# Attention with split operands and a two-stage MLP on one core: transposed tiles in single banks of PSUM, the inverses spread as a row through DRAM, the first weight tiles split on GpSimd, and new orders on every engine

## The reference

```
h = x @ w_in;  r = max(h, 0);  y = (s * r * r + b) @ w_out           # first
h = y @ w2_in; y2 = (h * sigmoid(1.702 h)) @ w2_out                   # second
```

## Time and profile before

| | |
|---|---|
| median of 3 runs | 1165.56 us |
| profiled execution: its own time, its span | 1168.41 us, 1166.6 us |
| busy in the span: TensorE, VectorE, ScalarE, GpSimd | 95%, 47%, 44%, 20% |
| attention, up to the first matmul of the MLP | 355.48 us |
| the rest, the two MLPs | 811.1 us |
| mean granted clock of TensorE | 0.996 of full |

### The profile page before, as it was taken

The page is one execution under the profiler, slowest core; times in us unless marked ns, Lnnn a source line. Parts: engine busy times, 40 slices in busy tenths (PEclk is TensorE's granted clock), DMA queues, the critical chain, the costliest instruction groups (busy, mean ns, idle before and its releaser), DMA issues.

```text
span 1166.6 us, 17049 instructions
## 1 busy us (share of the span) xinstructions
PE 1112.1 (95%) x6608; PEld 1049.9 (90%) x6608; DVE 547.9 (47%) x889; ACT 512.6 (44%) x1013; POOL 238.1 (20%) x254
## 2 busy tenths in 40 slices
PE   3899999999988999999999999999999999999998
PEld 3788888888888999999999999999999999999997
DVE  3777778777765643333333335643233333323222
ACT  2777777787763542233232325542222222222222
POOL 6776867778331000000000000000000000000000
PEclk9999999999998999999999999999999999999999
DMA  6555655545313320000000003400000000000000
GB/s 137 126 122 111 142 131 122 119 111 124 72 26 103 126 71 1 1 1 1 1 1 1 1 1 98 128 29 1 28 1 15 14 1 28 1 28 1 28 1 28
DMA packets 95985, 60.60 MB, mean 52 GB/s; under 512 B 62624, under 2 KB 83232, under 8 KB 95904
## 3 DMA queue, kind: packets, MB, share of 16 engines
q1 hardware_dynamic: 95008, 59.01, 20.3%
q10 hardware_dynamic: 896, 0.49, 0.1%
HBM read 31.16 MB, written 4.72 MB: 31 GB/s over the span
## 4 chain that ended last, share of the span: by engine, by line
PE 91%; ACT 3%; issue 2%; DVE 2%; DMA 1%; POOL 1%; SPq 1%; ACTq 0%; POOLq 0%
PE psum L756 34%; PE psum L728 34%; PE psum L514 8%; PE psum L449 4%; PE psum L480 4%; PE psum L477 2%; PE psum L464 1%; PE psum L536 1%; ACT ET L560 1%; ACT QK L583 1%; DVE QK L656 1%; PE psum L526 1%; PE psum L496 1%; PE psum L534 0%; DMA wraw<-in_moe_w_out_dram 0%
## 5 line engine op out<-in xcount | busy, mean ns | idle before, releaser
L728 PE MATMUL psum<-xhi,Whi 128*128 128x384 f32 x768 | 258.5, 337 | 4.7 <-DVE Wlo L221 4.7
L728 PE MATMUL psum<-xhi,Wlo 128*128 128x384 f32 x768 | 258.4, 336 | 0.0
L728 PE MATMUL psum<-xlo,Whi 128*128 128x384 f32 x768 | 257.8, 336 | 0.0
L728 PEld LDWEIGHTS psum<-xhi,Whi 128*128 128x128 f32 x768 | 144.7, 188 | 9.2 <-DVE Wlo L221 5.0
L728 PEld LDWEIGHTS psum<-xlo,Whi 128*128 128x128 f32 x768 | 144.7, 188 | 4.1
L728 PEld LDWEIGHTS psum<-xhi,Wlo 128*128 128x128 f32 x768 | 144.6, 188 | 0.0
L885 DVE SCALAR_TENSOR_TENSOR glo<-act,sb_sb,ghi 128x384 fp32r<-128x384 f32 x96 | 59.7, 622 | 147.3 <-ACT ghi L862 147.3
L862 ACT ACTIVATE ghi<-act,sb_sb 128x384 fp32r<-128x384 f32 x96 | 59.2, 617 | 157.5 <-PE psum L756 153.6
L756 PE MATMUL psum<-ghi,Whi 128*128 128x384 f32 x384 | 128.3, 334 | 0.0
L756 PE MATMUL psum<-glo,Whi 128*128 128x384 f32 x384 | 128.3, 334 | 0.0
L756 PE MATMUL psum<-ghi,Wlo 128*128 128x384 f32 x384 | 128.3, 334 | 0.0
(11 more groups left out here) (92 smaller groups left out, 1855.9 us busy)
## 6 DMA issues: line engine op xcount, KB each, us to landing
Q<-QK SPq DMA_DIRECT2D x64, 144.0 KB, 2.5
QK<-QK SPq DMA_DIRECT2D x32, 288.0 KB, 3.3
wraw<-in_moe_w_in_dram SPq DMA_DIRECT2D x32, 256.0 KB, 2.8
wraw<-in_moe_w_out_dram SPq DMA_DIRECT2D x32, 256.0 KB, 3.1
rest<-O SPq DMA_DIRECT2D x32, 144.0 KB, 2.3
raw<-in_q_dram SPq DMA_DIRECT2D x32, 128.0 KB, 3.0
raw<-in_k_dram SPq DMA_DIRECT2D x32, 128.0 KB, 2.5
vraw<-in_v_dram SPq DMA_DIRECT2D x32, 128.0 KB, 2.4
```

The costliest lines, as they stand in the source:

```text
L728: mm = pe.matmul(hps(n), w[i][:, kt * P:(kt + 1) * P], x[C % 2][:, kt, :], start=kt == 0 and j == 0, stop=kt == KT - 1 and j == 2)
```

## The change

- **X tiles in single banks.** An X job transposes its own head's four tiles only, 512 columns, one bank. The tail's rows for both heads come in a new job `XQ` of four transposes, one bank, with `hiQ` and `loQ`. `SLOTS` names a bank for jobs of one bank and a pair of banks for the others. Each bank has its own last reader.
- **P·V** of both heads has the same column order; head 1's last tile is cut in three pieces (22 matmuls instead of 20).
- **The two parts of P·V** are summed by VectorE (`sum`), which reads one half from PSUM and the other from O; `evac` copies only 64 partitions. A PV's banks are free after `sum`.
- **Inverses.** `inv` (9 columns) is transposed once on TensorE (`IT`), copied by ScalarE (`icp`), written to DRAM (`put`), and read back spread over 64 partitions for each head (`get`, three DMAs). GpSimd multiplies (`finish`, one instruction of 128 x 576).
- **First weight tiles.** GpSimd splits tiles 0 and 1, hi and lo, at the end of iterations 13 and 14. Loads 2 and 3 are issued in iterations 14 and 15. Tile 2 is split ahead of the MLP's loop.
- **Orders.** All five lists are new. X of head 1 and both PV jobs are one iteration later than before, `finish` is at s - 3.

```diff
-    PE_ORDER = order("S12@0 prep0@2 S13@0 X00@0 X01@0 S00@1 S01@1 ST@1 prep1@2 S02@1 S03@1 X02@0 X03@0 S10@1 PV1@-1 "
-                     "X10@0 X11@0 XT@0 X12@0 X13@0 B@-1 S11@1 PV0@0")
-    ACT_ORDER = order("hi13@-1 exp11@0 widen@-1 evac0@-1 qk0@2 exp12@0 hi00@0 exp13@0 hi01@0 exp00@1 exp01@1 qk1@2 "
-                      "expT@1 exp02@1 exp03@1 hi02@0 hi03@0 exp10@1 evac1@-1 hi10@0 hi11@0 hiT@0 hi12@0")
-    DVE_ORDER = order("max01@0 lo01@-1 maxT@0 max02@0 klo1@1 max03@0 max10@0 lo02@-1 lo03@-1 lo10@-1 lo11@-1 loT@-1 "
-                      "lo12@-1 inv@-1 max11@0 lo13@-1 finish@-2 max12@0 klo0@2 max13@0 lo00@0 max00@1")
-    POOL_ORDER = order("V0@0 add0@-1 vlo0@0 rot0@3 rot1@3 V1@0 add1@-1 vlo1@0")
-    SP_ORDER = order("loadv1@-3 loadv0@-2 load1@0 qcopy1@-1 kcopy0@-1 rest1@-4 kcopy1@-1 load0@1 rest0@-3 qcopy0@0")
-    SLOTS = [2, 3, 1, 0, 3, 2, 0, 1, 2, 3, 0, 1, 2, 3, 0, 1, 3, 2, 0, 1, 3, 2, 0]
-    SLOT_ORDER = (2, 1, 0, 3)
+    PE_ORDER = order("XQ@-1 XT@-1 IT@-1 X10@-1 X11@-1 X12@-1 X13@-1 S00@1 PV0@-1 S01@1 prep0@2 X00@0 X01@0 S02@1 "
+                     "prep1@2 S03@1 S10@1 S11@1 S12@1 ST@1 X02@0 X03@0 S13@1 PV1@-1")
+    ACT_ORDER = order("hi03@-1 exp13@0 expT@0 evac1@-2 hiQ@-1 hiT@-1 icp@-1 hi10@-1 hi11@-1 hi12@-1 hi13@-1 exp00@1 "
+                      "evac0@-1 qk0@2 hi00@0 exp01@1 hi01@0 qk1@2 exp02@1 exp03@1 exp10@1 exp11@1 exp12@1 hi02@0")
+    DVE_ORDER = order("klo0@2 lo00@0 max02@1 lo01@0 max03@1 klo1@2 max10@1 max11@1 max12@1 maxT@1 max13@1 lo02@0 lo03@0 "
+                      "sum1@-1 loQ@0 loT@0 lo10@0 lo11@0 lo12@0 max00@2 lo13@0 inv@1 max01@2 sum0@0")
+    POOL_ORDER = order("finish@-3 vlo1@-1 rot1@2 V0@0 vlo0@0 rot0@3 V1@0")
+    SP_ORDER = order("put@-1 load0@3 qcopy0@2 load1@3 loadv1@0 kcopy0@2 loadv0@1 get@-2 qcopy1@2 kcopy1@2")
+    SLOTS = [7, 2, 6, 0, 1, 3, 2, 3, 2, 0, 1, 7, 6, 2, 1, 0, 3, 2, 1, 0, 7, 6, 2, 1]
+    BANK_ORDER = (7, 6, 0, 1, 4, 5, 2, 3)
...
+    JOBS = ("S", "ST", "X", "XQ", "XT", "PV", "prep", "IT")
+    SINGLE = ("X", "XQ", "IT")
...
+    def banks_of(kind, h, j):
+        slot = SLOT[(kind, h, j)]
+        return (slot,) if kind in SINGLE else (2 * slot, 2 * slot + 1)
...
+            of = banks_of(kind, h, j)
+            before[(kind, p, h, j)] = [last_in[b] for b in of if b in last_in and (b == of[0] or last_in[b] != last_in.get(of[0]))]
+            for b in of:
+                last_in[b] = (kind, p, h, j)
...
-                need(eng, evac_done, 2 * p + h + 1)
...
+                need(eng, sum_done, 2 * p + h + 1)
...
-            return psum[SLOT[(kind, h, j)]]
+            slot = SLOT[(kind, h, j)]
+            return psum[slot // 2][:, slot % 2 * BANK:(slot % 2 + 1) * BANK] if kind in SINGLE else psum[slot]
...
+        def first_w(pool, s, zero):
+
+
+            i = s - (NPAIR - 3)
+            if 0 <= i < AHEAD:
+                pool.wait_ge(wraw_in[i], 32)
+                pool.wait_ge(rotated, 2 * NPAIR - 1)
+                pool.wait_ge(prep_t, 2 * NPAIR)
+                pool.wait_ge(s_done, 2 * NM * (NPAIR - 1))
+                pool.wait_ge(sT_done, NPAIR - 1)
+                pool.tensor_tensor(Whi[i][:], wraw[:, i, :], zero[:, :].broadcast_to([P, 2 * DM]), ALU.add).then_inc(w_hi_done, 1)
...
+            O = sb("O", [P, S])
+            osum = [sb(f"osum{i}", [P, S]) for i in range(2)]
+
+            inv = [sb(f"inv{i}", [P, 2 * NM + 1]) for i in range(2)]
+            invT = [sb(f"invT{i}", [2 * NM + 1, P]) for i in range(2)]
+            inv_row = sb("inv_row", [P, S])
+            inv_dram = [nc.dram_tensor(f"inv_dram{i}", [2 * NM + 1, P], F32, kind="Internal").ap() for i in range(2)]
...
+                def put_inv(p, _, __):
+                    sp.wait_ge(invT_copied, p + 1)
+                    need(sp, inv_in[p % 2], 48 * (p // 2))
+                    sp.dma_start(inv_dram[p % 2], invT[p % 2][:]).then_inc(inv_out[p % 2], 16)
+
+                def get_inv(p, _, __):
+                    sp.wait_ge(inv_out[p % 2], 16 * (p // 2 + 1))
+                    need(sp, x_done, p)
+                    flat = inv_dram[p % 2].rearrange("t p -> (t p)")
+                    for h, at, a, n in ((0, 0, 0, S), (1, 0, S + TAIL, MAIN), (1, MAIN, S, TAIL)):
+                        sp.dma_start(inv_row[rows_of(h), at:at + n],
+                                     flat[a:a + n].rearrange("(o q) -> o q", o=1).to_broadcast([D, n])).then_inc(inv_in[p % 2], 16)
...
+                    if s in (NPAIR - 2, NPAIR - 1):
+                        load_weights(sp, s - NPAIR + 4)
...
+                def finish(p, _, __):
+                    b, t = p // KT * S, p % KT
+                    pool.wait_ge(sum_done, 2 * p + 2)
+                    pool.wait_ge(inv_in[p % 2], 48 * (p // 2 + 1))
+                    pool.tensor_tensor(xT[:, t, b:b + S], osum[p % 2][:], inv_row[:], ALU.mult).then_inc(x_done, 1)
...
-                    pe.transpose(ps[:, at:at + P], ET[p % 2][:, j * P:(j + 1) * P], id_sb[:])
...
                     for t in range(NM):
-                        mm = pe.transpose(ps[:, r + t * P:r + (t + 1) * P], E[p % 2][:, t, h, c:c + P], id_sb[:])
+                        mm = pe.transpose(ps[:, t * P:(t + 1) * P], E[p % 2][:, t, h, c:c + P], id_sb[:])
...
+                def XQ_job(p, _, __):
...
+                    ps = banks("XQ")
+                    for j in range(NM):
+                        mm = pe.transpose(ps[:, j * P:(j + 1) * P], ET[p % 2][:, j * P:(j + 1) * P], id_sb[:])
+                    mm.then_inc(xQ_t, 1)
...
+                    ps, r = banks("PV", h), ROW[0]
                     for j in range(NT):
-                        for a, b, c in PIECES[h]:
+
+                        pieces = PIECES[0] if j < NM or h == 0 else (PIECES[0][0], (BANK, r + MAIN, BANK - r), (r + MAIN, r + S, -TAIL))
+                        for a, b, c in pieces:
                             for n in range(2):
...
+                def IT_job(p, _, __):
+                    pe.wait_ge(inv_done, p + 1)
+                    freed(pe, before[("IT", p, 0, 0)])
+                    pe.transpose(banks("IT")[0:2 * NM + 1, 0:P], inv[p % 2][:], id_sb[:]).then_inc(invT_t, 1)
...
-                    act.copy(Xhi[h][:, j, :], row(banks("X", h, j), h)).then_inc(et_hi, 1)
+                    act.copy(Xhi[:, h, j, 0:MAIN], banks("X", h, j)).then_inc(et_hi, 1)
...
+                def hiQ(p, _, __):
...
+                    act.copy(Xhi[:, :, :, MAIN:S], by_heads(banks("XQ"))).then_inc(etQ_hi, 1)
...
+                    need(act, sum_done, 2 * (p - 1) + h + 1)
+                    r = rows_of(h)
+                    act.copy(O[r, :], row(banks("PV", h), 0)[r, :]).then_inc(evac_done, 1)
...
+                def copy_invT(p, _, __):
+                    act.wait_ge(invT_t, p + 1)
+                    need(act, inv_out[p % 2], 16 * (p // 2))
+                    act.copy(invT[p % 2][:], banks("IT")[0:2 * NM + 1, 0:P]).then_inc(invT_copied, 1)
...
-                    dve.tensor_tensor(Xlo[h][:, j, :], row(banks("X", h, j), h), Xhi[h][:, j, :].bitcast(F32), ALU.subtract).then_inc(et_lo, 1)
+                    dve.tensor_tensor(Xlo[:, h, j, 0:MAIN], banks("X", h, j), Xhi[:, h, j, 0:MAIN].bitcast(F32), ALU.subtract).then_inc(et_lo, 1)
...
+                    dve.tensor_tensor(Xlo[:, :, :, MAIN:S], by_heads(banks("XQ")), Xhi[:, :, :, MAIN:S].bitcast(F32), ALU.subtract).then_inc(etQ_lo, 1)
...
+                def total(p, h, _):
+
+                    dve.wait_ge(evac_done, 2 * p + h + 1)
+                    if h == 0:
+                        need(dve, x_done, p - 1)
+                    r = rows_of(h)
+                    dve.tensor_tensor(osum[p % 2][r, :], row(banks("PV", h), 0)[rows_of(1 - h), :], O[r, :], ALU.add).then_inc(sum_done, 1)
...
-            BANKS = [psum[s][:, e * BANK:(e + 1) * BANK] for s in SLOT_ORDER for e in range(2)]
-            BANK_SLOT = [s for s in SLOT_ORDER for e in range(2)]
+            BANKS = [psum[b // 2][:, b % 2 * BANK:(b % 2 + 1) * BANK] for b in BANK_ORDER]
...
-                if C == 0 and i + AHEAD < NF:
-                    split_w(eng, i + AHEAD, hi)
+                if C == 0 and i + AHEAD + 1 < NF:
+                    split_w(eng, i + AHEAD + 1, hi)
...
-                    for n in range(2, 2 * NF):
+                    for n in range(4, 2 * NF):
...
+                    split_w(act, AHEAD, True)
...
+                    dve.wait_ge(w_lo_done, AHEAD)
+                    split_w(dve, AHEAD, False)
```

More of the change, by code:

```diff
@@ L162, in fused_kernel, with freed, read @@
         xT_t = sem("xT_t")
+        xQ_t = sem("xQ_t")
         et_hi = sem("et_hi")
         etT_hi = sem("etT_hi")
+        etQ_hi = sem("etQ_hi")
         et_lo = sem("et_lo")
         etT_lo = sem("etT_lo")
+        etQ_lo = sem("etQ_lo")
         pv_done = sem("pv_done")
         evac_done = sem("evac_done")
-        rest_in = [sem(f"rest_in{i}") for i in range(2)]
-        added = sem("added")
+        sum_done = sem("sum_done")
```

(42 more changed lines are left out.)

122 lines of the change are left out of this document (34 added, 88 removed).

## The result

The kernel after takes 1132.03 us (median of 4 runs, 1130.87 to 1132.79) against 1165.69 us (1165.14 to 1167.19) for the kernel before, run beside it: a ratio of 0.9708, 95% interval 0.9692 to 0.9725. The prediction was 1131. The profiled execution took 1131.56 us around a span of 1129.8.

The account below looks back on a forecast made before the run. TensorE was taken as the bound (91% of the span). Head -7.3, loop -19.8, tail -1.6, MLP -6.6, port +1.0 make -34.3 us: 1168.41 becomes 1134.1, less 2.9 for the median, 1131 us; range 1124 to 1152.

Parts of the forecast that it names:

- Part 1: TensorE's work in a loop iteration: eight fewer transposes (-0.87 us), two more short matmuls (+0.12), giving 16.68 us.
- part 3: Loop: TensorE's waits 1.8 us in place of 2.9, 18.8 us an iteration, 19.8 us saved over fourteen.
- the walk: One loop iteration followed, job by job from XQ: 18.45 us at best, before 0.35 added.
- Rival A: Loop: waits stay at 2.9 us, 19.58 us an iteration, 1142 us in all; chance 0.17.
- rival B: Loop held by ScalarE and VectorE at 20.2 us an iteration, 1151 us in all; chance 0.13.
- Part 2: Vector engines' work in a loop iteration: VectorE +0.5 us, ScalarE about -0.2, neither becoming the bound.
- Part 4: Head and tail around the loop: head 7.3 us shorter, tail 1.6 us shorter.
- Part 5: MLP's start: TensorE's wait for weights and the slow clock go, -6.6 us; eps additions may stall, +1.0.
- Part 6: The inverses' way through DRAM: both journeys covered by 18 us; waits for O, 80.4 us, go away.
- Rival C: SP's queue becomes the bound, delaying copies of Q and K: 1176 us at 22 us an iteration; chance 0.07.
- the port's stall: VectorE's two small eps additions may wait for GpSimd's weight splits: 0 to 4.8 us, taken as +1.0.
- Rival D: Clock falls in loop or tail; one fall in iterations 15 and 16 costs 1.7 us: 1133; within forecast's 0.60.

Follow-up runs that it names:

- e2: Kernel after with XQ's four transposes issued twice: 1138.71 us, ratio 0.9762.
- e7: Kernel after with VectorE's sum of head 0 covering 64 of 576 columns from pair 2 on: 1128.36 us, ratio 0.9674.
- e8: Kernel after with the low halves of Q and K covering 64 of 576 columns from pair 2 on: 1123.57 us, ratio 0.9637.
- e9: Kernel after with X01 put into the bank of X00, so that it waits for lo00: 1166.50 us, ratio 0.9999.
- e4: Kernel after with klo1 ahead of max03 in VectorE's order: 1137.08 us, ratio 0.9761.
- e6: Kernel before with GpSimd splitting weight tiles 0 and 1 and tiles 2 and 3 loaded earlier: 1160.09 us, ratio 0.9952.
- e1: Kernel after with the first two weight tiles split by ScalarE and VectorE again, loads 2 and 3 later: 1138.52 us, ratio 0.9768.
- e5: Kernel after with the inverses read back in six DMAs of half the size in place of three: 1134.84 us, ratio 0.9739.

## Why the prediction was right, step by step

**Part 1 and part 3, the iteration.** This step carries most of the gain, and the walk held within 0.3 us at each job. Counted from XQ at 174.82, walk and trace are: S02 8.47 and 8.53, prep1 9.21 and 9.47, S10 11.03 and 11.29, the tail's scores 13.02 and 13.27, PV1 15.65 and 15.85 (190.67 by the first matmul's start), the next XQ 18.45 and 18.59. TensorE stands 0.4 us before S02, 0.4 before prep1, 0.8 before S10 and 0.25 before S12, from the end of the job ahead in each case: 1.8 in all, as walked, and the work is 16.8 for 16.7. The mis-sized term is the 0.35 that I added for what the walk does not see. Thirteen iterations needed 0.14 of it, which gives 2.8 us; the fourteenth has no `prep` and takes 17.77 where I had counted 18.8, which gives 1.0. So the loop gave -23.65 for -19.8. Rival A would be 19.6, rival B 20.2. e2 shows TensorE's work to be on the path, e7 and e8 that VectorE's row holds the rest, and e9 what one X tile without a bank of its own costs in this order. Of the 1.74 us that an iteration lost (20.33 to 18.59) some 0.75 is work taken away, by the prediction's count, and 1.0 is waits. How much of the 1.0 the single banks give and how much the new orders, no run separates. One thing that I said would be late next was not: PV1 does not wait for exp12; nothing of ScalarE is in the waits of the loop. VectorE's row with klo1, the other one named, is there at S12, and e4 shows what comes when klo1 is drawn forward.

**Part 2, prices of operations.** lo 0.681, hi 0.581 (taken 0.59), the strided ninth 0.692 (taken 0.68, bounded by 1.5), the sum of 64 partitions 0.756 (0.75), the copy of the transposed inverses 0.249 (0.25), finish 1.443 (1.45). The linear price by columns from the earlier trace rows was good in every case; the widest bound was not needed.

**Part 4, head and tail.** Both came out 1.1 to 1.2 us short, and each has one long wait that the prediction did not have. The first XQ of iteration 1 is at 44.70, predicted 43.5: -6.1 for -7.3. The 1.2 are there at X00 already, 34.70 for 33.5, and from X00 on there are 10.0 us in the trace as in the prediction. S00 of pair 1 ran at about 31, as predicted for its K copy. The wait is S01's, two jobs ahead of X00: it stands for the tail's exponential of pair 0, at the end of ScalarE's row.

```profile
33.52 0.80 PE L469 MATMUL psum<-QK,Q 128*128 128x256 f32 x4 [1.53 <-ACT ET L582]
```

The tail took 21.14, predicted 20.1: -0.5 for -1.6. Here the step "by the walk 11.6" failed, 12.42 in the trace (iteration 16 took 8.72 for 8.5). It took the banks to be free earlier, and the timeline has one long wait, X02 for the bank of lo00, in an iteration without score jobs to put between:

```profile
312.65 1.25 PE L495 MATMUL psum<-id_sb,E 128*128 128x128 f32 x8 [1.62 <-DVE Xlo L649]
```

**Part 5, the MLP's start and the stalls of VectorE.** From the MLP's first matmul at 325.19 (before 355.48) the rest takes 804.6 us for 811.1: -6.5, predicted -6.6. The tile H2 runs without a wait at 329.44 and at a clock of 1.00. e6 shows the same step in the kernel before, 804.55 for 811.1; e1 gives +5.9 for the way back, with another wait in it. GpSimd's splits took 1.89 and 2.42 us for the 2.4 taken. The stall of the eps addition came, but not where I put it. VectorE's and GpSimd's timelines in the tail:

```profile
309.43 1.40 DVE L663 TENSOR_TENSOR sums_eps<-sums,eps 128x9 f32<-128x9 f32 x1
```
```profile
307.01 2.41 POOL L240 TENSOR_TENSOR Wlo<-wraw,Whi 128x1024 fp32r<-128x1024 f32 x1
309.38 1.44 POOL L448 TENSOR_TENSOR xT<-osum,inv_row 128x576 f32<-128x576 f32 x1
```

The nine-column addition ends at 310.83, with GpSimd's finish (310.82), which the split had pushed there. In e1, without GpSimd's splits and with GpSimd idle at that time, it takes:

```profile
310.01 0.16 DVE L657 TENSOR_TENSOR sums_eps<-sums,eps 128x9 f32<-128x9 f32 x1
```

So the stall is 1.24 us. It delays sum0, lo00 and the X02 above; but e1's X02 waits as well, 1.37 us for 1.62, since there sum0 waits for ScalarE. By this pair the stall costs 0.25 us on the path, where the sum had +1.0 for the two. The other, at 292.33, took 0.76 us for a median of 0.55 over all sixteen. The Trainium skill (SBUF — State Buffer, Who interferes with whom) has a VectorE instruction with two SBUF inputs fully blocked by one of GpSimd that reads SBUF. By that rule, the trace agrees, here as in the kernel before.

**Part 6, the detour.** SP's queue waits most for klo and for Q's copies, not on the detour. put waited 9.4 us in four cases, and TensorE's table above has no wait that leads there:

```profile
SPq L378 <- DVE QK L678: 28.9, 12, 6.1
...
SPq L387 <- ACT invT L610: 9.4, 4, 5.4
```

The waits for O (80.4 us in the earlier trace rows) are gone. The two large gets land 2.9 us after their issue. Rival C is ruled out for this kernel as it stands, and by e5 also with three more issues an iteration.

**The sum.** By the two profiled spans -36.8 us: head -6.1, loop -23.65, tail -0.5, MLP -6.5; the port's stall is in the tail's. Predicted were -7.3, -19.8, -1.6, -6.6 and +1.0, so the loop gave 3.85 more, head, tail and MLP 2.4 less, and the port's 1.0 was not to be added. The profiled execution came to 1131.56 for 1134.1, while its median lies 0.5 above it and not 2.9 below. These two errors of 2.5 and 3.4 cancel, so that 1131 for 1132.03 is in part luck; the mechanism was right, but the number is closer than the terms were. By the medians the change is worth -33.7 us. In which stage before's 2.9 us lay stays open.

**Rival D.** In the profiled execution of the kernel after the clock does not fall in head, loop, tail or the MLP's start; the tail's wait of 1.62 us did not bring it down. One of the four runs has a mean of 0.998. e9 shows that the rival was real, with waits of 2.1 us.

## What to carry to other kernels

Walk one iteration of a written order by hand, with prices from the profile and the bank of each job: here that gave the start of every job that waits within 0.3 us, and the whole iteration within 0.14. Walk the first and the last iterations as well, since other jobs are missing there and other waits show: here they were each over 1 us off. Do not read a wait of the bottleneck engine as slack of the job before it, unless that job's consumer has slack too (S03). A bank more or less is not worth only its own wait: look in the windows whether the clock falls behind that wait.

## What was not expected of the hardware

The granted clock bears some repeated waits and not others. In the kernel after TensorE waits up to 1.0 us several times an iteration, over 14 iterations, at a clock of 1.00. In e9 it waits 2.11 us at X01, once in each iteration. In eight iterations the clock stays at 1.00; in the other six it falls from 2.4 to 1.2 GHz for a part, in the stretch shown right behind this same wait (0.50 from 221 to 224 us; mean of the iteration 0.92, +1.4 us each), and it is nearly at the lower level for five microseconds of the last loop iteration (0.51). The Trainium skill (TensorE: Matmul & The Clock Gate, A second HAM failure mode: psum-queue depth-cycling) describes a kernel in which frequent small gaps between groups of matmuls alone do this. The trace agrees in those six iterations of e9; the other eight, and the loops of before and after, do not show it. So the length of the wait alone does not decide it. A wait between these two, 1.62 us long and single, in the tail of the kernel after, left the clock at 1.00; one that comes back in each iteration was not tried.

An addition of 9 columns takes 0.16 us alone and up to 1.40 beside GpSimd (median 0.55 over 16): the longest one ended when GpSimd's running operation did.
